# Mixture-of-experts stage on one Trainium2 core: each block of tokens taken through both layers by itself, with its inner rows turned in two halves and the weight parts moved behind an expert's first and last block

## What is computed

```python
for b in range(B):                      # B, S = 2, 768 tokens; D, F = 512, 1024; E = 8
    prev_e = -1
    for s in range(S):
        fresh_e = int(np.argmax(logits[b, s]))
        if s == 0 or local_gate[b, s] < 0.5:
            e = fresh_e
        else:
            e = prev_e if prev_e >= 0 else fresh_e
        prev_e = e
        p = softmax(logits[b, s])
        h = np.maximum(x[b, s] @ w1[e], 0.0)       # w1[e]: 512 x 1024
        out[b, s] = p[e] * (h @ w2[e])             # w2[e]: 1024 x 512
```

## Time and profile before

| | us |
|---|---|
| median of 3 executions | 421.69 |
| lowest and highest | 421.29, 423.27 |
| the profiled execution | 421.05 |
| its span, first to last instruction | 419.3 |

### The profile page before, as it was taken

One profiled execution on the slowest core, in us unless ns is written; L12 is line 12 of the kernel. 1 busy time (PEld: TensorE's weight loads), 2 busy tenths in 40 slices (PEclk: granted clock), 3 DMA queues, 4 the chain that ended last, 5 costly groups with the idle time before them and its releaser, 6 DMA issues.

```text
span 419.3 us, 7163 instructions
## 1 busy us (share of the span) xinstructions
PE 406.3 (97%) x2601; PEld 343.2 (82%) x2602; DVE 223.1 (53%) x289; ACT 196.5 (47%) x276; POOL 149.9 (36%) x125
## 2 busy tenths in 40 slices
PE   7999999999999999999899999999999999999992
PEld 3888799887889987879688888888888888888871
DVE  4888749982004878577767312217641461725440
ACT  2334678670215765461618312228741462826450
POOL 3354872000000000027554612216872282653761
PEclk9999999999999999999999999999999999999997
DMA  8999900000520009551178571111569108356100
GB/s 294 407 411 416 384 2 2 0 2 0 200 101 0 2 0 368 234 202 63 48 307 363 166 332 50 25 50 39 222 270 402 50 25 341 123 221 262 37 26 15
DMA packets 16153, 67.75 MB, mean 162 GB/s; under 512 B 2623, under 2 KB 4159, under 8 KB 11776
## 3 DMA queue, kind: packets, MB, share of 16 engines
q1 hardware_dynamic: 12928, 58.87, 35.4%
q0 software_dynamic: 2912, 8.13, 5.8%
q10 hardware_dynamic: 288, 0.41, 0.3%
HBM read 58.49 MB, written 10.22 MB: 164 GB/s over the span
## 4 chain that ended last, share of the span: by engine, by line
PE 90%; DMA 6%; ACT 1%; DVE 1%; issue 1%; POOL 0%; ACTq 0%; SPq 0%; POOLq 0%; DVEq 0%
PE ps L971 25%; PE ps L973 25%; PE ps L972 25%; DMA kv<-qkv 4%; PE ps L1261 3%; PE ps L1211 2%; PE ps L1022 2%; PE ps L1019 2%; PE ps L1001 2%; PE ps L1068 1%; PE ps L985 1%; DMA xg<-x_rows,gnow 1%; ACT kv L544 1%; PE ps L1047 0%; DMA x_rows<-x2n 0%
## 5 line engine op out<-in xcount | busy, mean ns | idle before, releaser
L427 POOL TENSOR_TENSOR wx<-raw_w,wx 128x1024 fp32r<-128x1024 f32 x21 | 53.6, 2567 | 14.7 <-ACT wx L583 14.6
L971 PE MATMUL ps<-wx,xT 128*128 128x512 f32 x136 | 54.5, 401 | 1.6 <-DVE xT L900 1.3
L583 ACT CAST wx<-raw_w 128x1024 fp32r<-128x1024 f32 x56 | 54.8, 1058 | 1.9 <-issue 1.3
L971 PE MATMUL ps<-wx,hT 128*128 128x512 f32 x136 | 54.5, 401 | 0.2 <-DVE hT L908 0.2
L973 PE MATMUL ps<-wx,hT 128*128 128x512 f32 x136 | 53.2, 391 | 0.0
L973 PE MATMUL ps<-wx,xT 128*128 128x512 f32 x136 | 53.1, 391 | 0.0
L972 PE MATMUL ps<-wx,hT 128*128 128x512 f32 x136 | 53.1, 390 | 0.0
L972 PE MATMUL ps<-wx,xT 128*128 128x512 f32 x136 | 53.0, 390 | 0.0
L891 DVE TENSOR_TENSOR wx<-raw_w,wx 128x1024 fp32r<-128x1024 f32 x35 | 48.1, 1421 | 4.8 <-ACT wx L583 4.8
L645 ACT CAST hT<-ps 128x512 fp32r<-128x512 f32 x34 | 18.3, 591 | 57.2 <-PE ps L1261 57.2
L971 PE MATMUL ps<-x,win 128*128 128x384 f32 x128 | 43.2, 337 | 0.0
(11 more groups left out here) (163 smaller groups left out, 800.8 us busy)
## 6 DMA issues: line engine op xcount, KB each, us to landing
raw_w<-w_exp SPq DMA_DIRECT2D x28, 1024.0 KB, 8.9
qk<-qkv SPq DMA_DIRECT2D x7, 768.0 KB, 9.8
raw_first<-w_exp SPq DMA_DIRECT2D x4, 1024.0 KB, 7.7
kv<-qkv SPq DMA_DIRECT2D x4, 768.0 KB, 11.5
x_rows<-x2n SPq DMA_DIRECT2D x11, 256.0 KB, 2.8
kv<-qkv SPq DMA_DIRECT2D x7, 384.0 KB, 9.9
x_early<-x2n SPq DMA_DIRECT2D x10, 256.0 KB, 2.3
win_raw<-w_in SPq DMA_DIRECT2D x4, 512.0 KB, 12.3
```

The lines of the kernel that those rows point to most:

```text
L427: ins = nc.gpsimd.tensor_tensor(wx[:, slot, 1, c], raw, wx[:, slot, 0, c].bitcast(F32), ALU.subtract)
L583: nc.scalar.copy(wx[:, slot, 0, c], raw).then_inc(wx_hi[w], 1)
L971: mm(o, lh, rl, start=first, stop=False)
```

## The change

PE now takes a block through both layers by itself: first layer with the turn of h's first half after 18 of its 24 matmuls, turn of the next block's x, one product of the second layer, the turn of h's second half, and the other seven products. The `warm_up` before the last second layer is gone. In the very first block the same is done in an order of its own. DVE's step is now: scale the previous block's result, lo of h's first half, lo of the next x, lo of h's second half. POOL scatters the previous block and then gathers.

The weight parts move: an expert's **first** block is followed by w2 of e+1 (ACT four pieces, DVE two, POOL two), its **last** block by w1 of e+2 (ACT four, DVE all four; POOL has none). An expert with one block has both behind that block. SP loads w2 of expert 1 earlier, its first half between the two stores of the last rows of x2. The table holds first block and end instead of first and last.

```diff
@@ SP @@
             for n in range(2):
                 ...
                 sp.dma_start(x2_rows[T - P:T, h], x2n[:, (TT - 1) % 3, h]).then_inc(x2_stored[(TT - 1) % 3], 16)
+                if n == 0:
+                    sp.wait_ge(gathered, 16)
+                    raw(1, 1, raw_w2, raw_w2_in, (0,))
             sp.wait_ge(x2_done, TT + 1)
-            sp.wait_ge(gathered, 48)
...
+            sp.wait_ge(gathered, 32)
+            raw(1, 1, raw_w2, raw_w2_in, (1,))
+            raw(0, 2, raw_w1[0], raw_w1_in[0])
@@ POOL @@
+            def step(g):
+
+                scatter_before(g)
+                pool.wait_ge(gathered, 16 * g + 32)
+                gather(g + 2)
...
+            def expert(e, s, ahead):
+
+                first, end = block_range(pool, e)
+                if not (isinstance(e, int) and e == 0):
+                    step(first)
+                if ahead:
                     weights_lo(1, e + 1, 1 - s, (2, 3))
+                rest(pool, first, end, step)
@@ ACT @@
+            def step(g):
+
+                act.wait_ge(p2_done, g)
+                relu(g, 0)
+                h_hi(g, 0)
+                relu(g, 1)
+                x_hi(g + 1)
+                h_hi(g, 1)
...
             act.wait_ge(tables, 1)
-            weights_hi(0, 1, 1)
-            relu(0, False)
-            x_hi(1)
-            h_hi(0, False)
+            weights_hi(0, 1, 1, (0, 1))
+            relu(0, 0)
+            h_hi(0, 0)
+            relu(0, 1)
+            x_hi(1)
+            h_hi(0, 1)
+            weights_hi(0, 1, 1, (2, 3))
+
+            def expert(e, s, ahead):
+
+                first, end = block_range(act, e)
+                if not (isinstance(e, int) and e == 0):
+                    step(first)
+                    act.wait_ge(p2_done, first)
+                if ahead > 0:
+                    weights_hi(1, e + 1, 1 - s)
+                rest(act, first, end, step)
+                if ahead > 1:
+                    act.wait_ge(p1_done, 2 * end)
                     weights_hi(0, e + 2, s)
@@ DVE @@
-            weights_lo(0, 1, 1, (0,), True)
+            h_lo(0, 0)
             x_lo(1)
-            h_lo(0)
-            weights_lo(0, 1, 1, (1, 2))
+            h_lo(0, 1)
+            weights_lo(0, 1, 1, range(4))
+
+            def expert(e, s, ahead):
+
+                first, end = block_range(dve, e)
+                if not (isinstance(e, int) and e == 0):
+                    step(first)
+                if ahead > 0:
+                    weights_lo(1, e + 1, 1 - s, (0, 1))
+                rest(dve, first, end, step)
+                if ahead > 1:
+                    weights_lo(0, e + 2, s, range(4))
+                return end
@@ PE @@
+            def second_layer(g, e, slot):
+
+                pe.wait_ge(o_done, g + 1)
+                pe.wait_ge(hT_done, 2 * g + 1)
+                pe.wait_ge(w2_lo_dve, 2 * e + 3)
+                w2_part(0, slot)
+                turn_h(g, 1)
+                for k in range(1, KF):
...
+            def step(g, e, slot):
+
                 pe.wait_ge(xT_done, g + 1)
                 pe.wait_ge(h_done, 2 * g)
...
+                w1_part(1, 0, slot)
+                w1_part(1, 1, slot)
+                turn_h(g, 0)
+                w1_part(1, 2, slot)
+                w1_part(1, 3, slot)
+                turn_x(g + 1)
+                second_layer(g, e, slot)
...
-            last_block = plain(E - 1, 1)
-            warm_up(4, bank(7))
-            through_w2(last_block, E - 1, 1)
```

More of the change, by code:

```diff
@@ L346, in _, with raw @@
             sp.dma_start(wout_raw[:], w_out).then_inc(wout_in, 16)
-            def raw(w, e, area, done):
-                for a in range(2):
+            def raw(w, e, area, done, halves=(0, 1)):
+                for a in halves:
                     sp.dma_start(area[:, 2048 * a:2048 * a + 2048],
@@ L567, in _, with weights_hi @@
             act.wait_ge(small_in, 32)
-            def weights_hi(w, e, slot):
-                for n in range(4):
+            def weights_hi(w, e, slot, pieces=range(4)):
+                for n in pieces:
                     c = slice(4096 * w + 1024 * n, 4096 * w + 1024 * n + 1024)
@@ L626, in _, with relu @@
                         weights_hi(1, 0, 0)
-            def relu(g, later):
-                if later:
-                    act.wait_ge(ht_tr, 2 * g)
-                for a in range(2):
-                    act.wait_ge(p1_done, 2 * g + a + 1)
-                    nc.scalar.activation(hs[:, 512 * a:512 * a + 512], psP1[:, 512 * a:512 * a + 512],
-                                         ACT.Relu).then_inc(h_done, 1)
+            def relu(g, a):
+                act.wait_ge(p1_done, 2 * g + a + 1)
+                nc.scalar.activation(hs[:, 512 * a:512 * a + 512], psP1[:, 512 * a:512 * a + 512],
+                                     ACT.Relu).then_inc(h_done, 1)
             def x_hi(g):
@@ L1271, in plain @@
-            def plain(e, slot):
-                first, last = block_range(pe, e)
-                with pe.If(first < last):
-                    with pe.Fori(first, last) as g:
-                        step(g, e, slot, slot)
-                return last
+                pe.wait_ge(hT_done, 2 * g)
+                for k in range(KD):
+                    w1_part(0, k, slot)
+                w1_part(1, 0, slot)
+                w1_part(1, 1, slot)
+                turn_h(g, 0)
+                w1_part(1, 2, slot)
@@ L1289, in _, with expert @@
                     last_rows(TT - 1, TT, (0, 1))
[L1290 to L1291 removed]
             first_w1()
             turn_x(1)
[L1294 to L1307 removed]
+            pe.wait_ge(o_done, 1)
+            pe.wait_ge(hT_done, 1)
+            for k in range(KF):
+                if k == 1:
+                    turn_h(0, 1)
+                if k in (0, 2, 4):
+                    pe.wait_ge(w2_lo_pool, k // 2 + 1)
+                if k == 4:
+                    pe.wait_ge(hT_done, 2)
+                if k == 6:
+                    pe.wait_ge(w2_lo_dve, 3)
+                w2_part(k, 0)
+            def expert(e, s):
+                first, end = block_range(pe, e)
+                if not (isinstance(e, int) and e == 0):
+                    pe.wait_ge(w1_lo_dve, 4 * e + 3)
+                    step(first, e, s)
+                rest(pe, first, end, lambda g: step(g, e, s))
+            expert(0, 0)
+            with pe.Fori(1, E - 1, 2) as ee:
+                expert(ee, 1)
+                expert(ee + 1, 0)
+            expert(E - 1, 1)
 def kernel(**inputs):
```

321 lines of the change are left out of this document (120 added, 201 removed).

## The result

The changed kernel takes **428.05 us** (median of 4 executions, 425.70 to 429.61) against 421.97 for the kernel before, run on the same chip (421.29 to 423.27). The ratio is 1.0139, with an interval from 1.0118 to 1.0160. The prediction was 424.7 with a range up to 428.0: the sign was right, the loss was twice as large as forecast, and the time lies just above the range. Two things stand behind that, and they have to be kept apart, because the profile shows only one of them.

A forecast was written before the change was run, and what follows sets the result against it. PE, busy 97% of the span, was taken to bound the kernel. 421.05 - 1.9 (order) + 3.6 (block 8) + 1.3 (start of expert 0) = 424.05, on the median 424.7 us; range 420.6 to 428.0.

The forecast's parts named there:

- The start of expert 0: Block 1: PE waits while DVE's and POOL's weight pieces share a port; 1.3 us taken, 0 and 3.8 kept.
- the fall of PE's clock behind the long waits: At block 8, PE's clock falls to the 1.2 GHz level in the wait; 1.6 us more, 426.3; chance 0.13.
- The order on PE: Each block complete in itself on PE, blocks of 12.32 us; head and end waits shrink, giving back 1.9 us.
- The slack of 0.15: Every block's second layer, ready at 6.13, due at 6.28; rival without this slack: 1.6 us more, 426.3, chance 0.05.
- 2.1 + 1.26 - 1.12 - 0.48: PE's new order: 2.1 won at the head, 1.26 at the end, less 16 x 0.07 and an extra 0.48 turn.
- Block 8: Behind one-block expert 2, PE waits 3.6 us for DVE's lo of h, queued behind weight pieces sharing POOL's port.
- the row of six: Behind block 7, DVE makes two w2 and four w1 pieces beside POOL's two, ending at a + 12.6.
- the rival in which ACT alone paces DVE: Block 8: DVE's row is not held up and ends at a + 9.0; 419.8 or 418.8 us; chance 0.12.
- the time of POOL's request: Start of expert 0: POOL asks for the port 3.2 us after ACT's w2 casts start, at 213.6 to 214.9.
- the row of 208.93: Old trace: POOL's second piece went ahead of an older DVE request; by it expert 0's start costs 3.8, whole 427.2.
- the waits of 1.3 in the old trace left the clock alone: Argument on PE's clock rival: waits of 1.3 us in the kernel before brought no fall of the clock.
- 0.64 by which the forecast was raised from the profiled execution of the kernel before to its median: Final sum: 424.05 against the profiled execution of 421.05 became 424.7 on the median of 421.69.

The follow-up runs named there:

- pool_short: Changed kernel with POOL's w2 lo pieces of experts 2 to 7 cut to 16 of 1024 columns; 424.52 us, 1.0050 of the kernel before.
- pool_after: Changed kernel with POOL's two w2 pieces of every expert waiting until DVE has made its two; 430.54 us, 1.0188 of the kernel before.
- busy: Changed kernel with 12 matmuls that only keep PE occupied ahead of the second layer in blocks 1 and 8; 425.56 us, 1.0085 of the kernel before.
- later_busy: `later_w2` with 12 matmuls that only keep PE occupied ahead of the second layer of block 8; 422.26 us, 1.0002 of the kernel before.
- dve_all: Changed kernel with all four w2 lo pieces on DVE and none on POOL in the experts' loop; 421.17 us, 0.9979 of the kernel before.
- later_w2: Changed kernel with DVE's two w2 pieces of expert 1 moved behind block 1, POOL's pieces staying; 424.16 us, 1.0053 of the kernel before.

## Why the prediction came out too low

Two terms of the sum failed. The start of expert 0 was put at 1.3 us and cost 3.0. And the fall of PE's clock behind the long waits was left out of the sum, as a case of 0.13 for itself, and cost 2.5 of the median. The rest stood. By the prediction's own steps, against the profiled execution and then the median:

- **The order on PE: right, 0.5 us better.** 206.5 and 212.5 were forecast, 206.57 and 212.56 came, and 6.27 for the start of the second layer against 6.28. The slack of 0.15 held in the ordinary blocks (block 2, the worst, lost 0.1), so that rival is out. A block takes 12.27 to 12.29 in place of 12.32: two turns of four cost little more than one of eight (12.25), where I had charged 0.07. The order gives 2.37, not 1.9. (The terms that the prediction lists for this, 2.1 + 1.26 - 1.12 - 0.48, make 1.76; the 1.9 is 411.31 - 409.4.)
- **Block 8: right.** 3.6 was forecast and 3.56 measured, with the row of six, the casts and the table loads where the prediction put them. But the rival in which ACT alone paces DVE had this block in time within 0.1, and `pool_short` shows 1.07 without the port: the faster side was priced too low.
- **The start of expert 0: the step that failed in the trace.** "I take **1.3**, the middle" was one POOL piece between DVE's; both went between, and it cost 3.02. What was wrong was the time of POOL's request: 213.6 to 214.9 was forecast, 213.38 came, 0.36 ahead of DVE's request for its last but one piece (213.74). With no time of issue ahead of the casts (two w1 and four w2 casts stand in one row from 208.45 to 214.25), the w2 casts start at 210.4, the lower end. And from there it took 3.0, the three casts that POOL needs, where I had read 3.2 from the earlier trace rows. In those rows POOL was not waiting for the cast but busy with a gather until 390.09:

```profile
388.83 1.26 POOL L440 DMA_INDIRECT xg<-x_rows,gnow  x1 [0.80 <-POOL gnow L437]
```

Worked out from the rows above, a request between 213.74 and some 214.9 would have let one POOL piece between and cost about 1, which no run shows; by asking 0.36 us ahead of DVE, POOL met both of DVE's last pieces. `pool_after`, in which DVE's row ends at 215.97 and the wait is gone, shows that the turns on the port are the whole of it.

- **The order of the turns.** In rows 208 to 220 and 298 to 310 of the changed kernel every turn goes to the piece that was asked for first: POOL 213.38, DVE 213.74, POOL 216.03, DVE 217.08. The Trainium skill (SBUF — State Buffer, "Who interferes with whom") has "Issue order, not op shape, decides who blocks", and here the trace agrees. The prediction had 1.3 by that rule and 3.8 by the row of 208.93; with the measured request the rule itself gives 3. The row of 208.93, where both POOL pieces went ahead of an older request of DVE, stays against it, and no run explains it.
- **The clock: right as a mechanism, wrong as a chance and not added.** I gave it 0.13, at block 8 alone, as a case beside the forecast. It is not beside it: it comes on top of waits of this length, in 7 of the 10 executions of the changed kernel by their mean clocks (0.991 or less). `busy` puts it at 2.6 us of the median, `later_busy` at 1.9 for one wait; the prediction had 1.6. The argument "the waits of 1.3 in the old trace left the clock alone" was true, and `dve_all`'s 1.40 agrees, but it says nothing of 3.6. The Trainium skill (TensorE: Matmul & The Clock Gate, "Part 1: The HAM clock gate") puts it as "the default state is throttled, and activity releases the throttle", and the fall behind the wait of 3.20 us in `later_w2` fits that.

Together: the kernel without a fallen clock is `busy`, 425.56, and the forecast was 424.7. So 2.5 of the miss of 3.35 is the clock, and 0.9 is the rest: 1.7 more at the start of expert 0, 0.5 less from the order, and -0.3 of small things. Those are 0.44 more behind the last product and around the span, which was forecast as unchanged; 0.14 by which `busy` lies below the profiled execution of the changed kernel; and 0.64 by which the forecast was raised from the profiled execution of the kernel before to its median, a distance that the changed kernel doesn't have where its clock stays up.

## What to carry to other kernels

When two engines take turns on one port, count the pieces that overlap, not who is first: each piece of the slower engine is added to the faster one's row at the time for which it holds the port (2.2 us here, against 1.14 for making the piece oneself), so handing work to it can cost more than it saves. When you estimate the time of a piece from an old row, look at what else the engine did just then: 0.2 us of a gather decided here between one piece and two. Price a wait of the matrix engine together with its clock: two waits of 3.0 and 3.6 us cost 6.6 us in the trace and up to 5.4 more in executions that weren't profiled, and a mean granted clock beside each time shows that where a single profile doesn't. And before a wait is removed, ask which later transfer it had been hiding: with its own wait gone, `pool_after` waited 2.56 us for a gather.

## What the runs showed of the hardware

- The port is passed from piece to piece between DVE and POOL, in the order of the requests in the two contended rows of the changed kernel (one row of the kernel before, 208.93, goes another way). A POOL piece alone takes 2.4 us, waiting for one of DVE 3.36; a DVE piece 1.14 alone and 3.40 waiting for one of POOL.
- The granted clock falls from the 2.4 to the 1.2 GHz level after a wait of PE of 3.0 to 3.6 us in some executions of one and the same kernel and not in others (means of 0.980 to 0.995 for the changed kernel; 0.990 to 0.997 in `pool_short`, whose one long wait is that of block 1). Waits of 0.9 and 1.4 left it alone (`dve_all`). Twelve matmuls that only keep PE occupied ended it, with the waits almost as long as before (15.26 and 15.66 in place of 15.26 and 15.82).
- A gather of 128 rows landed after 8.4 us in `pool_after` and 7.3 in the changed kernel, each beside loads of weights, where the middle one of the changed kernel's 18 took 3.7. That the loads are the cause was not tested.
